# One core, attention followed by two feed-forward layers: the reciprocal kept in PSUM, and the order of an attention pair changed

## What is computed

```python
def _attn_ref(q, k, v, alpha):            # each (4, 8, 768, 48)
    for t in range(S):
        state = alpha[:, :, t, :, None] * state + np.einsum('bhd,bhe->bhde', k[:, :, t], v[:, :, t])
        y[:, :, t] = np.einsum('bhd,bhde->bhe', q[:, :, t], state)
    return y
```

## Time and profile before

| | |
|---|---|
| three runs | 848.61 us median (847.53 to 849.88) |
| the profiled execution | 854.97 us, span 853.2 us |
| busy share of the span | PE 93%, DVE 83%, ACT 71%, POOL 37% |
| attention, from the first load to the last copy of y | 1.3 to 181.6 us |
| DMA of the whole span | 42.95 MB, most of it in packets under 512 B |

### The profile page before, as it was taken

How to read it: one execution, slowest core, us unless ns; L and a number is a source line. 1 busy time by engine, 2 the same in 40 slices (tenths; PEclk the granted TensorE clock), 3 DMA queues, 4 the chain that set the end, 5 groups by cost and what they waited for, 6 DMA issues and landing times.

```text
span 853.2 us, 16078 instructions
## 1 busy us (share of the span) xinstructions
PE 794.8 (93%) x5298; PEld 735.9 (86%) x5298; DVE 712.0 (83%) x1263; ACT 604.3 (71%) x1226; POOL 315.4 (37%) x376
## 2 busy tenths in 40 slices
PE   3898889968998999999999999999999999999986
PEld 3676767757888999999999999999999999999975
DVE  4899999938999898888988889888889888988642
ACT  3667667827887788677877768876778777787522
POOL 6999987001222333232332223332323233233201
PEclk9989999989999999999999999999999999999998
DMA  8889878610000001001000100010001000000000
GB/s 187 199 199 224 207 169 194 149 57 28 1 28 2 1 10 39 10 1 37 9 9 9 37 0 9 9 37 9 0 9 37 9 9 1 10 10 10 10 10 28
DMA packets 113173, 42.95 MB, mean 50 GB/s; under 512 B 101616, under 2 KB 110960, under 8 KB 113136
## 3 DMA queue, kind: packets, MB, share of 16 engines
q1 hardware_dynamic: 110336, 33.04, 16.4%
q0 software_dynamic: 2800, 9.45, 3.8%
HBM read 33.04 MB, written 9.44 MB: 50 GB/s over the span
## 4 chain that ended last, share of the span: by engine, by line
PE 59%; DVE 10%; ACT 6%; issue 2%; DMA 1%; DVEq 0%; POOL 0%; ACTq 0%; SPq 0%
PE h_ps L893 17%; PE acc_ps L909 16%; PE y_ps L875 12%; PE z_ps L928 12%; PE z_ps L938 2%; DVE work L1123 2%; DVE rec L1115 2%; DVE den L1111 2%; ACT rec L1012 1%; ACT g_hi L1008 1%; DVE den L1128 1%; ACT rec L1014 1%; DVE solu L1087 1%; DVE work L1131 1%; ACT den L985 1%
## 5 line engine op out<-in xcount | busy, mean ns | idle before, releaser
L1066 POOL TENSOR_TENSOR g_lo<-work,g_hi 128x384 fp32r<-128x384 f32 x128 | 130.5, 1020 | 409.4 <-ACT g_hi L1008 409.4
L893 PE MATMUL h_ps<-x,w 128*128 (+1 forms) x1152 | 226.9, 341 | 7.2 <-DVE work L1133 4.4
L909 PE MATMUL acc_ps<-g_hi,w 128*128 128x384 f32 x768 | 218.3, 338 | 2.3 <-POOL g_lo L1066 2.3
L893 PEld LDWEIGHTS h_ps<-x,w 128*128 128x128 f32 x1152 | 202.1, 188 | 15.3 <-DVE work L1133 11.7
L909 PEld LDWEIGHTS acc_ps<-g_hi,w 128*128 128x128 f32 x768 | 141.2, 188 | 2.8 <-POOL g_lo L1066 2.8
L982 ACT ACTIVATE h<-h_ps 128x384 f32<-128x384 f32 x128 | 61.6, 482 | 100.1 <-PE h_ps L893 100.1
L909 PE MATMUL acc_ps<-g_lo,w 128*128 128x384 f32 x384 | 129.6, 338 | 0.0
L875 PE MATMUL y_ps<-w,lnT 128*128 128x384 f32 x576 | 111.5, 344 | 2.7 <-DVE ysb L1154 2.7
L1128 DVE SCALAR_TENSOR_TENSOR den<-h,ncoef,den 128x384 f32<-128x384 f32 x128 | 78.7, 615 | 41.0 <-ACT den L985 40.1
L875 PEld LDWEIGHTS y_ps<-w,lnT 128*128 128x128 f32 x576 | 104.5, 192 | 4.9 <-DVE lnT L1145 3.0
L928 PE MATMUL z_ps<-w,x 128*128 128x512 f32 x414 | 104.3, 397 | 3.3 <-DVE lnT L1145 3.3
(11 more groups left out here) (113 smaller groups left out, 1169.8 us busy)
## 6 DMA issues: line engine op xcount, KB each, us to landing
chunks_ain<-in_alpha_dram SPq DMA_DIRECT2D x32, 144.0 KB, 3.2
chunks_xin<-in_q_dram SPq DMA_DIRECT2D x32, 144.0 KB, 2.7
chunks_xin<-in_k_dram SPq DMA_DIRECT2D x32, 144.0 KB, 2.9
wstage<-in_moe_w_in_dram POOLq DMA_DIRECT2D x9, 512.0 KB, 5.3
chunks_vin<-in_v_dram SPq DMA_DIRECT2D x16, 288.0 KB, 3.8
attention_out<-chunks_yout SPq DMA_DIRECT2D x32, 144.0 KB, 3.0
x<-attention_out SPq DMA_DIRECT2D x8, 576.0 KB, 3.8
out_dram<-ysb SPq DMA_DIRECT2D x24, 192.0 KB, 1.8
```

Source lines behind the costliest of these rows:

```text
L893: mm = nc.tensor.matmul(h_ps[s % 2][:, 0:TT], w1[:, wz, kc, s * P:(s + 1) * P], xs[:, xz, kc, :], start=(n == 0), stop=(n == 3 * KC - 1))
L909: mm = nc.tensor.matmul(acc_ps[:, dc, 0:TT], w2[:, wz, f, dc * P:(dc + 1) * P], rhs, start=(f == 0 and n == 0), stop=(f == FC1 - 1 and n = ...
L1066: nc.gpsimd.tensor_tensor(g_lo[:, 1 - o, :], gate[:, 1 - o, :], g_hi[:, 1 - o, :].bitcast(F32), ALU.subtract).then_inc(glo_done, 1)
```

## The change

In the attention alone:

- Once `qp` is made, ScalarE writes the first reciprocal into the PSUM tile `turn_aq` instead of `rec`, and VectorE reads it there for `err` and `rec`. So alpha of the next pair can be turned only when `rec` is done; its turn moves to the end of TensorE's iteration, and it signals after three and after six transposes.
- `ktv` is gone. The products of `ktok` and v are made for six chunks instead of five and are written to y with a step, so that the state scan reads them straight from PSUM, as (state + product) * end of b. `bstep` holds five ends instead of four, a zero in the sixth place starts each new row, and `kp` is transposed for six chunks.
- The mask of chunks 4 and 5 stands in front of `err`.
- ScalarE's squares of q and k are two instructions, one before and one after the reciprocal's exponential; `bstep` comes first.
- SP loads q and k of pair n before alpha of pair n + 1, and GpSimd begins with the weights only when the first k is in.

```diff
...
-        bstep = sb("bstep", [P, 2, D, NC - 1])
-        ktok = sb("ktok", [P, NC - 1, ROWS])
...
-        ktv = sb("ktv", [P, D, NC - 1])
...
@@ -186,17 +185,18 @@
 
                 def body(n, o, i):
 
+                    if stage1(n):
+                        for x, src, turned, squared in ((Q, q, q_turned, qsq_seen), (K, k, k_turned, ksq_seen)):
+                            if not i_is(n, 0):
+                                wait_alone(sp, turned, n, carrier)
+                                wait_alone(sp, squared, n, carrier)
+                            load_heads(xin[:, x], src, n, x_loaded[x])
                     if stage1(n + 1):
                         if not i_is(n, 0):
-                            wait_alone(sp, a_turned, n, carrier)
+                            wait_alone(sp, a_turned, n * 2, carrier)
                             wait_alone(sp, range_seen, n * 2, carrier)
                         load_heads(ain[:, 1 - o], alpha, n + 1, a_loaded[1 - o])
...
-                        for x, src, turned in ((Q, q, q_turned), (K, k, k_turned)):
-                            if not i_is(n, 0):
-                                wait_alone(sp, turned, n, carrier)
-                                wait_alone(sp, xsq_seen, n, carrier)
...
+                pool.wait_ge(x_loaded[K], 32)
                 prepare_weights(pool)
 
             @block.tensor
             def _(pe):
-                def turn(src, out, done):
+                def turn(src, out, done, each=NC):
                     for c in range(NC):
                         mm = nc.tensor.transpose(out[0:ROWS, c // CPH, (c % CPH) * P:(c % CPH + 1) * P],
                                                  src[:, c, :], ident[:])
-                    mm.then_inc(done, 1)
+                        if c % each == each - 1:
+                            mm.then_inc(done, 1)
 
                 def attention_products(p, chunks):
 
...
-                        for c in range(NC - 1):
+                        for c in range(NC):
...
-                        for c in range(NC - 1):
+                        for c in range(NC):
                             for j in range(2):
                                 wide = HB if j == 0 else D
-                                mm = nc.tensor.matmul(y[j * HB:j * HB + wide, 1, c * D:(c + 1) * D],
+                                mm = nc.tensor.matmul(y[j * HB:j * HB + wide, 1, 0:D * NC].rearrange("p (e c) -> p e c", c=NC)[:, :, c],
...
-                    if stage1(n + 1):
-                        pe.wait_ge(a_loaded[1 - o], (i + o + 1) * 32)
-                        pe.wait_ge(qp_ready, n + 1)
-                        turn(ain[:, 1 - o], turn_aq, a_turned)
-                    if stage2(n):
                         for c in range(CPH):
                             within(p, c)
                         pe.wait_ge(st_ready, n)
...
                         mm.then_inc(y_done, 1)
+                    if stage1(n + 1):
+                        pe.wait_ge(a_loaded[1 - o], (i + o + 1) * 32)
+                        pe.wait_ge(rec_done, n + 1)
+                        turn(ain[:, 1 - o], turn_aq, a_turned, CPH)
...
+                                             .rearrange("p (c d) -> p c d", c=NC - CPH), ACT.Copy).then_inc(ktok_ready, 1)
                     if stage1(n):
 
                         act.wait_ge(b_ready, n + 1)
+                        wait(act, st_ready, n - 1)
+                        nc.scalar.activation(bstep[0:ROWS, o, :, 0:NC - 1],
+                                             bp[0:ROWS, o, :].rearrange("p (c t) -> p c t", t=P)[:, 0:NC - 1, P - 1]
+                                             .unsqueeze(1).to_broadcast([ROWS, D, NC - 1]), ACT.Copy).then_inc(bstep_ready, 1)
                         wait(act, kp_ready, n)
                         nc.scalar.activation(rec[0:ROWS, :], bp[0:ROWS, o, :], ACT.Ln).then_inc(ln_done, 1)
+                        act.wait_ge(x_loaded[Q], n * 32 + 32)
+                        act.wait_ge(range_seen, n * 2 + 2)
+                        nc.scalar.activation(junk[:, 0:NC * ROWS], xin[:, Q].rearrange("p c d -> p (c d)"), ACT.Square,
+                                             accum_out=seen[:, 2, bass.ds(n, 1)]).then_inc(qsq_seen, 1)
                         act.wait_ge(ln_done, n + 1)
-                        nc.scalar.activation(rec[0:ROWS, :], rec[0:ROWS, :], ACT.Exp, scale=-1.0).then_inc(rec0_ready, 1)
-                        wait(act, st_ready, n - 1)
-                        nc.scalar.activation(bstep[0:ROWS, o, :, 1:],
-                                             bp[0:ROWS, o, :].rearrange("p (c t) -> p c t", t=P)[:, 1:NC - 1, P - 1]
-                                             .unsqueeze(1).to_broadcast([ROWS, D, NC - 2]), ACT.Copy).then_inc(bstep_ready, 1)
-
-                        for x in (Q, K):
-                            act.wait_ge(x_loaded[x], n * 32 + 32)
-                        act.wait_ge(range_seen, n * 2 + 2)
-                        nc.scalar.activation(junk[:], xin[:, Q:K + 1].rearrange("p x c d -> p (x c d)"), ACT.Square,
-                                             accum_out=seen[:, 2, bass.ds(n, 1)]).then_inc(xsq_seen, 1)
+                        act.wait_ge(qp_ready, n + 1)
+                        nc.scalar.activation(turn_aq[0:ROWS, :, 0:HS], halves(rec[0:ROWS, :]), ACT.Exp, scale=-1.0
+                                             ).then_inc(rec0_ready, 1)
+                        act.wait_ge(x_loaded[K], n * 32 + 32)
+                        act.wait_ge(qsq_seen, n + 1)
...
-                        dve.wait_ge(a_turned, n + 1)
+                        dve.wait_ge(a_turned, n * 2 + 1)
                         if not isinstance(n, int) or n >= 2:
                             dve.wait_ge(qp_ready, n)
-                            dve.wait_ge(ktv_ready, n - 1)
                             dve.wait_ge(bstep_ready, n)
                         for c in range(NC):
+                            if c == CPH:
+                                dve.wait_ge(a_turned, n * 2 + 2)
                             src = turn_aq[0:ROWS, c // CPH, (c % CPH) * P:(c % CPH + 1) * P]
                             last = nc.vector.tensor_tensor_scan(bp[0:ROWS, o, c * P:(c + 1) * P], src,
...
-                        wait(dve, y_done, n * 2 - 2)
                         nc.vector.tensor_tensor(halves(qp[0:ROWS, o, :]), turn_aq[0:ROWS, :, 0:HS], halves(bp[0:ROWS, o, :]),
                                                 ALU.mult).then_inc(qp_ready, 1)
                     if stage2(n):
 
                         dve.wait_ge(m_done, n)
-                        ends = bp[0:ROWS, p, :].rearrange("p (c t) -> p c t", t=P)[:, 0:NC - 1, P - 1]
-                        nc.vector.tensor_tensor(
-                            ktv[0:ROWS],
-                            y[0:ROWS, 1, 0:(NC - 1) * D].rearrange("p (c e) -> p e c", e=D),
-                            ends.unsqueeze(1).to_broadcast([ROWS, D, NC - 1]), ALU.mult).then_inc(ktv_ready, 1)
-
-                        dve.wait_ge(ktv_ready, n)
                         dve.wait_ge(bstep_ready, n)
                         nc.vector.tensor_tensor_scan(
-                            st[0:ROWS].rearrange("p e c -> p (e c)"), bstep[0:ROWS, p].rearrange("p e c -> p (e c)"),
-                            ktv[0:ROWS].rearrange("p e c -> p (e c)"), 0.0, ALU.mult, ALU.add).then_inc(st_ready, 1)
-                    if stage1(n):
-
-                        dve.wait_ge(rec0_ready, n + 1)
-                        nc.vector.tensor_tensor(err[0:ROWS, :], bp[0:ROWS, o, :], rec[0:ROWS, :], ALU.mult).then_inc(err_done, 1)
-                    if stage2(n):
+                            st[0:ROWS].rearrange("p e c -> p (e c)"), y[0:ROWS, 1, 0:D * NC],
+                            bstep[0:ROWS, p].rearrange("p e c -> p (e c)"), 0.0, ALU.add, ALU.mult).then_inc(st_ready, 1)
                         dve.wait_ge(att_done, n * 2)
                         mask(4, NC)
                     if stage1(n):
+
+                        dve.wait_ge(rec0_ready, n + 1)
+                        nc.vector.tensor_tensor(halves(err[0:ROWS, :]), halves(bp[0:ROWS, o, :]), turn_aq[0:ROWS, :, 0:HS],
+                                                ALU.mult).then_inc(err_done, 1)
                         dve.wait_ge(err_done, n + 1)
-                        nc.vector.scalar_tensor_tensor(out=rec[0:ROWS, :], in0=err[0:ROWS, :], scalar=2.0, in1=rec[0:ROWS, :],
-                                                       op0=ALU.subtract, op1=ALU.mult).then_inc(rec_done, 1)
+                        nc.vector.scalar_tensor_tensor(out=halves(rec[0:ROWS, :]), in0=halves(err[0:ROWS, :]), scalar=2.0,
+                                                       in1=turn_aq[0:ROWS, :, 0:HS], op0=ALU.subtract, op1=ALU.mult).then_inc(rec_done, 1)
                         dve.wait_ge(k_turned, n + 1)
                         dve.wait_ge(rec_done, n + 1)
```

37 lines of the change are left out of this document (20 added, 17 removed).

## The result

The changed kernel takes 836.96 us median (835.87 to 838.26, 4 runs), the kernel before on the same chip 848.5 us (847.53 to 849.88, 4 runs): ratio 0.9863, 95% interval [0.9843, 0.9883], a gain of 11.5 us. The forecast was 827.5, the range 820 to 836. The direction is right, the size is not. Its profiled execution took 838.26 us (span 836.5).

A forecast was written before the change was run, and what follows sets the result against it. Bound: VectorE held up by GpSimd, then TensorE at 9.05 us per period. Start -4.5, first period +1.8, periods -19.6, tail +0.2, DMA +1.0 make -21.1: 854.97 profiled to 833.9, less 6.4 gives 827.5 us; range 820 to 836.

The forecast's parts named there:

- the last of the sum: Whole kernel: from 833.9 us forecast for the profiled execution, 6.4 us subtracted to reach a median of 827.5.
- Start: Attention's first pair: earlier q and k loads and held weights bring pair 1's scans from 18.54 to 14.0, -4.5 us.
- slow first period: First period of the attention: TensorE is slow behind idle time, making that period 1.8 us longer.
- DMA: Loads and stores in the attention stage: tighter while weights load, 1.0 us allowed between 0 and 7.7.
- Rival 1: DMA bounds the attention while weights load: period 9.85 for some nine pairs, 834 to 836 us; chance 0.2.
- Absorbed: Attention loads: issued some 6 us before they are needed, so a DMA backlog of a few us costs nothing.
- The exclusion and its end: VectorE's two-SBUF-input instructions wait for GpSimd; one PSUM operand ends this, reciprocal step from 1936 to about 1000 ns.
- rival 4: TensorE's ktok products: writing y with a step of six elements is slow, 869 us at four times the length; chance 0.03.
- Rival 2: Attention periods: the chains interlock better and TensorE's pitch is less, period 8.6, 821 us; chance 0.12.
- rival 3: VectorE against GpSimd: the exclusion stays despite a PSUM operand, only the start is gained, 844 us; chance 0.03.
- hidden by only 0.2: ScalarE's reciprocal exponential ends at 5.9 us in the period, err wants it at 6.1, so it costs nothing.
- The PSUM operand: VectorE's err, rec and scan: reading one input from PSUM costs 0.06 us each, 0.18 per pair.

The follow-up runs named there:

- a_mask: Changed kernel with VectorE's second mask (chunks 4 and 5) put back behind err; 841.27 us, ratio 0.9887.
- a_sbuf: Changed kernel with the reciprocal written to and read from the SBUF tile rec again, order and waits as changed; 852.78 us, ratio 1.0014.
- b_again: Kernel before, unchanged, run and profiled a second time; 851.22 us median, 850.17 us profiled.
- b_onein: Kernel before with GpSimd's two-input subtraction made a one-input scaled copy, leaving out the weights' remainders; 842.23 us, ratio 0.9915.
- a_onein: Changed kernel with GpSimd's two-input subtraction made a one-input scaled copy, leaving out the weights' remainders; 836.83 us, ratio 0.9840.
- b_start: Kernel before with q and k loaded ahead of the next alpha and GpSimd waiting for the first k; 853.69 us, ratio 1.0032.
- a_core: Changed kernel with the old order of loads, no GpSimd wait for the first k, and the second mask behind err; 841.94 us, ratio 0.9891.
- a_nohold: Changed kernel without GpSimd's wait for the first k, so the weights' loads start at once; 835.23 us, ratio 0.9821.
- a_again: Changed kernel, unchanged, run and profiled a second time; 839.25 us, ratio 0.9864.
- a_thin: Changed kernel loading only half of each weight piece from the third on, GpSimd's instructions kept as long; 834.13 us, ratio 0.9808.

## Why the prediction missed

**The step that failed is the last of the sum: "the median of the three runs is 848.61, 6.4 lower, and 827.5 is what I give".** I subtracted the whole difference between one profiled execution and the median as if it were a constant of the measurement. The changed kernel's own profile was 838.26, only 1.3 above its median. That offset alone is 6.4 - 1.3 = 5.1 us of the miss. It is no constant: over the thirteen other profiles here, the profiled execution lies between 3.5 us below the median of its run (a_mask) and 4.4 above it (a_sbuf), and b_again's lies 1.05 below. In the first profile 4.8 us of it were that execution's start and periods, as b_again shows. My sum then also removed this ill luck: it took -4.5 from a start at 18.54 and -19.6 from periods of 146.3, where b_again has 16.84 and 143.2. Counted from that profile, 850.17, the same forecasts of the changed kernel's times give 850.17 - 21.1 + 4.8 = 833.9 with nothing to subtract behind it. So the 4.8 us were counted twice, once in the terms and once in the offset. (The other 1.6 of the 6.4 lie between b_again's profile and the 848.61; no run traces them.) The range had no term for the offset either; about 833.9 it would have held the result.

The other 4.4 us, from 833.9 forecast for the profile to 838.26 measured:

- *Start:* pair 1 at 14.57 instead of 14.0, 0.6. The slow first period is 11.09 instead of 9.05 + 1.8 = 10.85, 0.2.
- *DMA:* the 13 periods behind the first are 120.4 instead of 117.7, 2.8, where 1.0 was allowed: 1.8 more. Rival 1 is not what happened, though: most periods run at 9.03 with a DMA share of 0.99, and there is no row of nine periods at 9.85. The engines keep up on average, and single transfers come late by more than their lead: a store six times (7.0 us, 3.75 the longest), q or k three times (1.7 us together). "Absorbed" was right for the mean and wrong for the single late transfer. The case against rival 1, that no load was waited for, rested on one execution too: in b_again TensorE waits 1.7 us for a load of k at 22.26.
- *Second stage,* carried over unchanged: 673.5 instead of 671.6, 1.9 longer in this profile. The same code took 669.3 to 674.1 in the fourteen profiles; that scatter was not in the range.

0.6 + 0.2 + 1.8 + 1.9 = 4.5, and with 5.1 for the offset the way from 827.5 to 837.0 is told but for 0.1.

**What held.** The exclusion and its end: `rec` 954 ns against "about 1000", the scan of 288 elements 756 against 780, and a_sbuf, b_onein and a_onein show the cause from three sides. The period: 9.03 to 9.06 against 9.05 beside every width of weight piece (that it stays so once GpSimd is idle, no run shows), with TensorE, busy 8.86 of it, the fullest engine. The stepped write of rival 4: 24 products in 0.87 us against the 0.94 estimated for plain ones, no cost. Rival 2 (period 8.6) and rival 3 (844) did not come. ScalarE "hidden by only 0.2": VectorE never waits for it, and once the mask is behind `err`, it waits 0.80 at 125.01 (a_mask). Weights were to end near 146.5, and ended at 146.2.

**What the sum had too dear or too cheap in single parts.** The PSUM operand, 0.06 us each: in b_again, once GpSimd is idle, `err` with two SBUF inputs takes 0.93 (at 156.62) and `rec` 0.95 (at 158.07); with one of PSUM they take 0.945 and 0.954, at most 0.015 more. The Trainium skill ("VectorE: DVE Perf Modes", section on the TRN2 errata) gives the fixed cycles from which I had estimated 0.065 us and set beside the earlier trace rows; these two pairs, with one input of two in PSUM, do not bear that out. The start, -4.5 in the sum, is worth nothing in the kernel before (b_start). In the changed one the order of loads and GpSimd's wait together bring pair 1 forward by 2.3 us (16.60 in a_core, 14.32 in a_mask), 1.7 of it by the order (14.91 in a_nohold), and the two ratios, 0.9891 and 0.9887, don't tell them apart; the wait of GpSimd alone gives nothing.

**What stays open.** That executions of the kernel before differ by how VectorE falls into step with GpSimd is seen in two profiles; no run controlled it, and in the timed executions it can't be seen. How much of the gain is VectorE's hold itself and how much TensorE's clock, which stood at 0.93 over the 14 periods before and at 1.00 after, no run separates: a_sbuf brings back both (0.91), b_onein takes away most of both (0.99). Why b_start is not the same but slower (its longer time at the lower clock is seen, not tested), and what makes the first period 11 to 12 us, was not tried.

## What to carry to other kernels

Before a sum is made against a profiled execution, ask whether its length is the kernel's or its own: if it lies well above the median and the kernel has two engines that hold each other up, take the terms from a second execution, or forecast the new kernel's time from its own period, without carrying the offset over, and put the offset into the range. A VectorE instruction on the critical path with both inputs in SBUF can be freed from GpSimd by moving one input to PSUM, and only the instructions that still have two SBUF inputs go on being held (a_sbuf: `rec` 1768 ns, the scan 757). While GpSimd holds VectorE, work saved elsewhere (a start 3 us earlier, a shorter chain) showed as nothing in b_start and a_sbuf; once that is gone the order of the mask showed, in the periods at least.

## What was not expected of the hardware

- GpSimd's two kinds of instruction hold a VectorE instruction with two SBUF inputs differently. The two-input subtraction holds it to 0.15 us before its end (b_again, 33.42 to 35.79; the scan of 0.66 ends at 36.30). The one-input copy of 2.78 us holds it for about 0.9 us only (b_onein), the 768-wide one of 2.15 us for 0.7 (b_again: copy at 65.87, scan from 66.14 to 67.23). The Trainium skill ("SBUF — State Buffer", section on the two separate sides) has the pair of ports locked for the whole instruction; for the one-input copy the runs show otherwise.
- It goes both ways: GpSimd's copy at 36.72 in b_again took 3.06 us instead of 2.78, having started while VectorE's `err` was running (36.22 to 37.15); the copy at 24.11 did the same.
- TensorE's first products behind a wait took 2.08 us for 16 instructions at 15.11, against 1.16 in later pairs. The granted clock is 1.00 in that whole first period, so this row does not explain them, though 16 such products took 2.05 us in b_start at 40.36, where the clock fell to 0.50. Nor does it sort the first period's length, 11.07 to 12.05 us over nine profiles of the changed kernel and its variants: 11.80 in a_again with the clock at 0.50 from 14.3 to 21 us, 12.04 in a_thin with 1.00 throughout.
